# Attention and two feed-forward layers on one core: who splits w_in, and where tile 2's w_in products stand in the second step

## The chip, the core and the metric

The kernel runs on one core of one Trainium2 chip. The metric is the device time of one execution in microseconds (us), the median of several runs. In the profile PE is TensorE, DVE is VectorE, ACT is ScalarE, POOL is GpSimd and SP is SyncE, whose queue issues nearly all DMAs.

## The reference

Three layers follow each other on 1536 rows (2 batches of 768) of width 512 (8 heads of 64):

```python
# attention, per batch and head: 768 queries, the last 128 keys and 4 sink keys
scores = q @ k.T / 8
keep   = (key < 4) | ((0 <= query - key) & (query - key < 128))
x      = softmax(where(keep, scores, -1e9)) @ v          # heads side by side: [1536, 512]

# first layer, d_ff = 1024
h    = x @ w_in
solu = h * softmax(h)
ln   = (solu - mean(solu)) / sqrt(var(solu) + 1e-6) * g_ln
x    = ln @ w_out

# second layer, d_ff = 2048
y = relu(x @ w2_in) ** 2 @ w2_out
```

## The kernel before

**Numbers in two parts.** A product of two f32 matrices is made of three products of a rounded type (fp32r). Each operand is rounded ("hi"), what the rounding lost is kept as a second operand ("lo"), and PE sums hi x hi, hi x lo and lo x hi. So every matrix that PE multiplies is first rounded by one engine and split (raw minus hi) by one. For w_in these are `round_w_in(c)` and `split_w_in(c)` for its 4 chunks of 128 rows (128x1024 each, in w_raw, w_hi, w_lo); for w_out `round_w_out(first, last)` on ACT and `split_w_out(first, last)` on DVE for the 8 chunks of 128x512 (wo_hi, wo_lo), with the layernorm's gain g_col multiplied in. `WO_POOL` names the w_out chunks that POOL does all by itself (`split_w_out(i, k)`, three instructions), `WO_DVE` the others.

**Stage A** goes over 12 tiles of 128 rows (`NT`), in a software pipeline written out by hand: each engine has a function `step(t)` that lists its instructions in order, and the engines wait for each other's semaphores. In step t PE does the values of tile t+1 (`values`, `sink_values`: probabilities times v, in o_ps), the transposes of tile t's normalised hidden rows (`transpose_ln(t)`), the scores of tile t+2 (`score(t + 2, p)`, p = 0 to 3 for four pairs of heads), the w_in products of tile t+1 (`hidden(t + 1, first, last)`, 24 matmuls of 128x512 in h_ps), the w_out products of tile t (`project(t, first, last)`, 24 matmuls), and the transposes of probabilities (`transpose_p`, `transpose_sinks`) and of tile t-1's result (`transpose_x2`). Around them ACT copies and rounds from PSUM, and makes the exponentials (`softmax_exp`, `hidden_exp`); DVE masks (`merge`), takes the row maxima (`row_max`, `hidden_max`), normalises (`normalize_p`), gates and measures (`gate_and_norm`: u = h * e, bn_stats, variance), normalises the hidden rows (`normalize_hidden`) and makes the low parts (`split_xT`, `split_lnT`, `split_k`, `split_q`); POOL computes the inverse deviation (`inverse_std`), zeroes the triangular halves of the transposed probabilities (`halves`) that `values` reads, rounds the sink probabilities (`gather_sinks`) and prepares the sinks' values (`build_v_sink`, `split_v_sink`).

**The first tiles** are special, since all of w_in and w_out has to be split while they run. Tile 0's w_in products go by chunk: `hidden_0(c, False)` needs w_hi only, `hidden_0(c, True)` needs w_lo as well. `first_step()` is step 0; its w_out products are `project_0(with_low, first, last)`. Step 1 is `step(1)` with exceptions: `project_0(True, 3, C1)` for tile 0 and the scores of tile 3 stand ahead of `transpose_ln(1)`. `ln_parts(t)` says in which PSUM banks the transposes of the layernorm land: for tile 0 in w1_ps and o_ps, for all others in w1_ps and the two banks of h_ps, so that `hidden(t + 1, ...)` has to wait until these are read. `keep_warm` issues matmuls whose result is not used.

**Stage B** (from about 250 us) is the second layer in 3 blocks of 512 rows (`hidden2`, `project2`). Its weights are loaded over w_in's and w_out's raw copies: SP's queue waits for w_split, w_split_pool, wo_split and wo_split_pool ahead of the first such load (L372 to L376).

Of the kernel before, what the change touches and what calls it, by code (L numbers as in the profile page):

```python
# [27 lines left out]
NT = BATCH * TPB  # L28
# [7 lines left out]
WO_POOL = (6, 7)  # L36
# [93 lines left out]
def attention_moe_program(nc, qT, kT, v, w_in, w_out, g_ln, w2_in, w2_out, out):  # L130
# [6 lines left out]
    with ctx:  # L137
# [174 lines left out]
        def _(sp):  # L312
# [55 lines left out]
            for n in range(3, NT):  # L368
# [33 lines left out]
        def _(pool):  # L402
# [67 lines left out]

            def split_v_sink(b):

                low = slice(2 * SK, SKS)
                nc.gpsimd.tensor_copy(v_sink[0:SKS, b, :], v_sink_raw[0:SKS, b, :]).then_inc(v_sink_step, 1)
                pool.wait_ge(v_sink_step, 2 * b + 2)
# [24 lines left out]
            pool.wait_ge(w_rounded, 1)  # L500
            for half in range(2):
                cols = slice(half * BANK, (half + 1) * BANK)
                nc.gpsimd.tensor_tensor(w_lo[:, 0, cols], w_raw[:, 0, cols], w_hi[:, 0, cols].bitcast(F32), ALU.subtract
                                        ).then_inc(w_split_pool, 1)
            build_v_sink(0)
            split_v_sink(0)
# [34 lines left out]
        def _(act):  # L541
# [87 lines left out]
            def step(t, nxt=True):  # L629
# [3 lines left out]
                if t > 1:  # L633
                    copy_x2(t - 1)
                if t > 1 and t + 3 < NT:
                    round_q(t + 3)
                round_xT(n)
                if t == 1:
                    copy_x2(0)
                round_lnT(t)  # L640
                if t == 1:
                    round_q(4)
                if nxt:
# [9 lines left out]
                    bias(t + 2, 1)  # L653
                    if t + 3 < NT:
                        round_k(t + 3)
                    for h in range(HG, H):
                        softmax_exp(t + 2, h)
                    hidden_exp(n)
                    copy_pT(t + 2, 0)
                    copy_x2T(t - 1)  # L660
                    copy_pT(t + 2, 1)
                    if has_sinks(t + 2):
                        copy_sinksT(t + 2)

            def first_step():
# [4 lines left out]
                round_w_out(3, len(WO_DVE))  # L670
# [5 lines left out]
                round_lnT(0)  # L676
                bias(2, 1)
# [16 lines left out]

            bias(0, 0)
# [19 lines left out]
            copy_pT(1, 1)  # L715
            copy_sinksT(1)
# [664 lines left out]
```

## Time and profile before

| | us |
|---|---|
| runs (3) | 513.96, 513.05, 513.89 |
| median | 513.89 |
| profiled execution, time | 512.32 |
| profiled execution, span | 510.6 |
| PE busy | 493.1 (97%) |
| DVE busy | 281.1 (55%) |
| ACT busy | 212.2 (42%) |
| POOL busy | 103.6 (20%) |

The span is the time from the first to the last profiled instruction; the time of the same execution is 1.72 us longer. The profiled execution was not the median one. PE's clock has two levels, 1.2 and 2.4 GHz; "granted clock 0.50" in a stretch means that it ran at 1.2 GHz all along, 1.00 that it ran at 2.4.

### The profile page before, as it was taken

What the parts mean: (1) busy time and instruction counts of PE and PEld (TensorE: products, weight loads), DVE (VectorE), ACT (ScalarE), POOL (GpSimd) and SP (SyncE); (2) the same over time, 40 slices, a digit from 0 to 9 for tenths busy, and PEclk for the clock granted to TensorE, in tenths of its full rate; (3) what the DMA queues carried; (4) which work ended last, traced back from release to release, by engine and by line L of the source; (5) the groups of instructions that cost most, each with busy time, mean ns of one, the idle gap of its engine ahead of it and who ended that gap; (6) DMA issues with size and microseconds to landing.
All of it is one profiled execution on the core that took longest, in us unless ns stands there. A gap on an engine that the chain in (4) does not pass through costs nothing.

```text
span 510.6 us, 7209 instructions
## 1 busy us (share of the span) xinstructions
PE 493.1 (97%) x2676; PEld 400.1 (78%) x2676; DVE 281.1 (55%) x501; ACT 212.2 (42%) x556; POOL 103.6 (20%) x139
## 2 busy tenths in 40 slices
PE   7977899999999999999999999999999999999997
PEld 5656687888788888878877888888888888888885
DVE  3989688787788787674689334333222223222222
ACT  3756176565666656553354233232122122121121
POOL 4436204220021122072997000000000000000000
PEclk9999699999999999999999999999999999999999
DMA  8820312323121020006200000020000002000002
GB/s 248 279 64 21 126 43 104 114 74 122 46 61 45 22 62 1 22 1 225 105 0 1 1 0 1 0 82 0 0 0 0 0 0 83 0 1 0 1 0 83
DMA packets 12837, 26.04 MB, mean 51 GB/s; under 512 B 1608, under 2 KB 2632, under 8 KB 12296
## 3 DMA queue, kind: packets, MB, share of 16 engines
q1 hardware_dynamic: 12504, 25.39, 15.4%
q8 instruction: 18, 0.29, 0.2%
q10 hardware_dynamic: 304, 0.27, 0.2%
q14 instruction: 11, 0.09, 0.1%
HBM read 22.51 MB, written 3.15 MB: 50 GB/s over the span
## 4 chain that ended last, share of the span: by engine, by line
PE 86%; DVE 7%; ACT 3%; DMA 1%; issue 1%; POOL 1%; SPq 0%; DVEq 0%; POOLq 0%
PE score_ps L1306 25%; PE h_ps L1318 12%; PE w_ps L1165 12%; PE h_ps L1127 12%; PE wt_ps L1318 6%; PE w_ps L1318 6%; PE o_ps L1097 3%; PE score_ps L1068 2%; ACT prob L574 2%; PE wt_ps L1075 2%; PE wt_ps L1068 1%; PE h_ps L1155 1%; PE o_ps L1193 1%; DMA w2in<-w_in 1%; PE o_ps L1114 1%
## 5 line engine op out<-in xcount | busy, mean ns | idle before, releaser
L1306 PE MATMUL score_ps<-x2T_hi,w2in_hi 128*128 (+1 forms) x192 | 74.9, 390 | 0.0
L1306 PE MATMUL score_ps<-x2T_hi,w2in_lo 128*128 (+1 forms) x192 | 74.7, 389 | 0.0
L1306 PE MATMUL score_ps<-x2T_lo,w2in_hi 128*128 (+1 forms) x192 | 74.7, 389 | 0.0
L1005 DVE TENSOR_TENSOR e<-e 128x512 f32<-128x512 f32 x24 | 18.5, 771 | 81.7 <-ACT e L744 81.7
L1005 DVE TENSOR_TENSOR sq<-relu 128x512 f32<-128x512 f32 x24 | 17.5, 728 | 80.5 <-ACT relu L744 80.5
L744 ACT ACTIVATE relu<-score_ps 128x512 f32<-128x512 f32 x24 | 14.4, 598 | 92.1 <-PE score_ps L1306 92.1
L744 ACT ACTIVATE e<-score_ps 128x512 f32<-128x512 f32 x24 | 14.4, 600 | 87.4 <-PE score_ps L1306 87.3
L1306 PEld LDWEIGHTS score_ps<-x2T_lo,w2in_hi 128*128 128x128 f32 x192 | 36.1, 188 | 7.4
L1306 PEld LDWEIGHTS score_ps<-x2T_hi,w2in_hi 128*128 128x128 f32 x192 | 36.0, 188 | 7.5
L1306 PEld LDWEIGHTS score_ps<-x2T_hi,w2in_lo 128*128 128x128 f32 x192 | 36.0, 188 | 7.4
L574 ACT ACTIVATE prob<-sm,nbias 128x132 f32<-128x132 f32 (+1 forms) x96 | 37.9, 396 | 0.5
L1127 PE MATMUL h_ps<-w_hi,xT_hi 128*128 128x512 f32 x88 | 35.6, 404 | 1.8 <-DVE xT_lo L881 1.8
L1165 PE MATMUL w_ps<-wo_hi,lnT_hi 128*128 128x512 f32 x88 | 35.8, 407 | 1.2 <-DVE lnT_lo L876 1.1
L1165 PE MATMUL w_ps<-wo_lo,lnT_hi 128*128 128x512 f32 x88 | 35.3, 401 | 0.0
L1165 PE MATMUL w_ps<-wo_hi,lnT_lo 128*128 128x512 f32 x88 | 34.4, 391 | 0.0
L1127 PE MATMUL h_ps<-w_hi,xT_lo 128*128 128x512 f32 x88 | 34.4, 390 | 0.0
L1127 PE MATMUL h_ps<-w_lo,xT_hi 128*128 128x512 f32 x88 | 34.3, 390 | 0.0
L426 POOL CAST p_sink<-prob 128x64 fp32r<-128x64 f32 x10 | 3.8, 381 | 115.0 <-DVE prob L869 104.1
L536 POOL TENSOR_TENSOR w2in_lo<-w2in,w2in_hi 128x512 fp32r<-128x512 f32 x16 | 25.6, 1599 | 1.3
L593 ACT ACTIVATE e<-h_ps,nhmax 128x512 f32<-128x512 f32 x24 | 16.3, 685 | 22.6 <-DVE nhmax L821 22.6
L1127 PEld LDWEIGHTS h_ps<-w_hi,xT_hi 128*128 128x128 f32 x88 | 16.5, 188 | 6.4 <-issue 2.0
L1165 PEld LDWEIGHTS w_ps<-wo_hi,lnT_hi 128*128 128x128 f32 x88 | 16.6, 189 | 5.9 <-DVE lnT_lo L876 1.8
(178 smaller groups left out, 1143.9 us busy)
## 6 DMA issues: line engine op xcount, KB each, us to landing
w2in<-w_in SPq DMA_DIRECT2D x4, 1024.0 KB, 5.2
w2out<-w_out SPq DMA_DIRECT2D x8, 512.0 KB, 7.5
V<-v SPq DMA_DIRECT2D x12, 256.0 KB, 2.7
k_raw<-kT SPq DMA_DIRECT2D x20, 132.0 KB, 2.8
q_raw<-qT SPq DMA_DIRECT2D x20, 128.0 KB, 2.8
w2in<-w_in SPq DMA_DIRECT2D x4, 512.0 KB, 6.1
w2in<-w_out SPq DMA_DIRECT2D x2, 1024.0 KB, 10.8
out<-u SPq DMA_DIRECT2D x6, 256.0 KB, 2.0
```

Source lines behind the costliest of these rows:

```text
L536: nc.gpsimd.tensor_tensor(w2in_lo[:, :, fs], w2in[:, :, fs], w2in_hi[:, :, fs].bitcast(F32), ALU.subtract).then_inc(w2in_split, 1)
L574: nc.scalar.activation(prob[:, h, seen(n)], sm[:, h, seen(n)], ACT.Exp, bias=nbias[:, h:h + 1], scale=SCALE, accum_out=psum_row[:, h:h + 1 ...
L593: nc.scalar.activation(e[:, cols], h_ps[:, cols], ACT.Exp, bias=nhmax[:, :], scale=1.0, accum_out=hsum[:, half:half + 1]).then_inc(h_exped, 1)
L744: nc.scalar.activation(relu[f % 2], h2_ps[f % 2], ACT.Relu).then_inc(relu_ready, 1)
L1005: nc.vector.tensor_tensor(sq[f % 2], relu[f % 2], relu[f % 2], ALU.mult).then_inc(sq_ready, 1)
L1068: done = mm(bank, qs[rows], ks[rows], start=(i == 0), stop=(i == len(products) - 1))
L1075: last = nc.tensor.transpose(pT_ps[g][:, j * P:(j + 1) * P], prob[:, g * HG + j, main(n)], ident[:, :])
L1097: last = mm(o_ps[rows, cols], V[:, slot, h * D:(h + 1) * D], pT[:, g, j * P:(j + 1) * P], start=(g == 0 and part == 0 and i < 2), stop=(al ...
L1127: done = mm(h_ps[:, cols], xs[:, c, :], ws[:, c, cols], start=(c == 0 and k == 0), stop=(c == MC - 1 and k == 2))
L1165: done = mm(x2_ps[:, :], ls[:, k, :], ws[:, k, :], start=(k == 0 and i == 0), stop=(k == C1 - 1 and i == 2))
L1306: done = mm(h2_ps[f % 2], ws[:, c, fs], xs[:, c, bass.ts(blk, BLK)], start=(c == 0 and i == 0), stop=(c == MC - 1 and i == 2))
L1318: done = mm(y_ps[q], gs[f % 2][:, qs], ws[:, f, :], start=(f == 0 and i == 0), stop=(f == C2 - 1 and i == 2))
```

## The change

- `split_w_in`: POOL makes the low parts of chunks 0, 2 and 3 (before: 0), DVE that of chunk 1 (before: 1, 2, 3). `round_w_in(0)` goes from DVE to ACT. The low part of v_sink for batch 0 goes from POOL to DVE.
- `WO_POOL` is (7,), before (6, 7): chunk 6 of w_out is rounded by ACT and split by DVE.
- Tile 1's layernorm is transposed into w1_ps and o_ps as well (`EARLY = 2`), and PE's second step is written out: tile 2's w_in products stand ahead of `transpose_ln(1)`, with `project_0(True, 2, C1)` between them; 16 w_out products stand between the scores and the transposes of tile 3.
- The order of the first two steps of ACT and DVE is changed: among others, one w_out chunk instead of three is rounded ahead of `round_xT(1)`, `split_xT(1)` stands between the two `stats(0, ...)`, `normalize_p(2, 1)` ahead of `hidden_max(1, ...)`, and `split_w_out(2, 7)` ahead of `normalize_hidden(1)`. On PE `hidden_0(2, True)` and `hidden_0(3, True)` go ahead of `transpose_p(1, 0)`; 3 `keep_warm` products remain 3, in two places.

```diff
-WO_POOL = (6, 7)
+WO_POOL = (7,)
+EARLY = 2
 ln_parts(t):
-            if t == 0:
+            if t < EARLY:
                 return [(0, 4, w1_ps[:, :], 2), (4, C1, o_ps[:, :], 1)]
 SP, ahead of the first load of w2_in:
-                    sp.wait_ge(w_split, MC - 1)
-                    sp.wait_ge(w_split_pool, 2)
+                    sp.wait_ge(w_split, 1)
+                    sp.wait_ge(w_split_pool, 2 * (MC - 1))
 POOL:
-            pool.wait_ge(w_rounded, 1)
-            for half in range(2):
-                ...
+            def split_w_in(c):
+                pool.wait_ge(*((w_rounded, 2) if c == 2 else (w_rounded_act, c // 3 + 1)))
+                for half in range(2):
+                    ...
+            split_w_in(0)
             build_v_sink(0)
-            split_v_sink(0)
+            round_v_sink(0)
+            split_w_in(2)
+            split_w_in(3)
             round_q(2)
             round_k(2)
             halves(1, 0)
 ACT:
+            round_w_in(0)
             bias(0, 0)
...
+            hidden_exp(0)
             copy_sinksT(1)
-            hidden_exp(0)
             act.wait_ge(g_loaded, 16)
-            round_w_out(0, 3)
+            round_w_out(0, 1)
             first_step()
-            for t in range(1, NT - 2):
+            second_step()
+            for t in range(EARLY, NT - 2):
 ACT first_step():
-                round_w_out(3, len(WO_DVE))
+                round_w_out(1, 5)
...
                 round_lnT(0)
+                round_w_out(5, len(WO_DVE))
                 bias(2, 1)
...
-                hidden_exp(1)
                 copy_pT(2, 0)
                 copy_pT(2, 1)
+                hidden_exp(1)
                 copy_sinksT(2)
+            def second_step():                     # ACT
+                round_xT(2)
+                copy_earlier(3, 0)
+                copy_earlier(3, 1)
+                round_q(4)
+                copy_x2(0)
+                bias(3, 0)
+                softmax_exp(3, 0)
+                softmax_exp(3, 1)
+                round_lnT(1)
+                copy_earlier(3, 2)
+                copy_earlier(3, 3)
+                softmax_exp(3, 2)
+                softmax_exp(3, 3)
+                finish(1)      # bias(3,1), round_k(4), 4 exponentials, hidden_exp(2), copies: as in step()
 DVE:
-            round_w_in(0)
             merge(0, 1)
...
+            round_w_in(2)
             split_w_in(1)
-            round_w_in(2)
...
             row_max(1, 0)
+            split_v_sink(0)
             merge(1, 3)
...
             normalize_p(1, 1)
-            split_w_in(2)
-            split_w_in(3)
             hidden_max(0, 0)
...
-            gate_and_norm(0)
             first_step()
 DVE first_step():
+                gate(0, 0)
+                gate(0, 1)
+                stats(0, 0)
+                split_xT(1)
+                stats(0, 1)
+                variance(0)
                 merge(2, 0)
                 merge(2, 1)
                 normalize_hidden(0)
                 row_max(2, 0)
-                split_w_out(0, 1)
                 merge(2, 2)
                 merge(2, 3)
                 row_max(2, 1)
+                split_w_out(0, 1)
                 for part in range(2):
                     split_lnT(0, part)
-                split_w_out(1, 2)
                 normalize_p(2, 0)
                 split_q(3)
+                split_w_out(1, 2)
+                normalize_p(2, 1)
                 hidden_max(1, 0)
                 hidden_max(1, 1)
                 hidden_max_all(1)
-                normalize_p(2, 1)
-                split_w_out(2, 3)
-                gate_and_norm(1)
                 split_k(3)
+            def second_step():                     # DVE
+                gate(1, 0)
+                gate(1, 1)
+                stats(1, 0)
+                stats(1, 1)
+                variance(1)
+                split_xT(2)
+                split_w_out(2, len(WO_DVE))
+                normalize_hidden(1)
+                merge(3, 0)
+                merge(3, 1)
+                row_max(3, 0)
+                for part in range(2):
+                    split_lnT(1, part)
+                merge(3, 2)
+                merge(3, 3)
+                row_max(3, 1)
+                normalize_p(3, 0)
+                split_k(4)
+                split_q(4)
+                hidden_max(2, 0)
+                hidden_max(2, 1)
+                hidden_max_all(2)
+                normalize_p(3, 1)
+                gate_and_norm(2)
 PE:
             hidden_0(0, True)
             hidden_0(1, True)
-            transpose_p(1, 0)
-            keep_warm(3)
-            transpose_p(1, 1)
             hidden_0(2, True)
             hidden_0(3, True)
+            transpose_p(1, 0)
+            keep_warm(1)
+            transpose_p(1, 1)
+            keep_warm(2)
             first_step()                           # its last project_0(True, 0, 3) is (True, 0, 2)
+            def second_step():                     # PE
+                values(2, 0)
+                values(2, 1)
+                sink_values(2)
+                score(3, 0)
+                score(3, 1)
+                pe.wait_ge(u_ready, 3)
+                hidden(2, 0, 12)
+                pe.wait_ge(u_ready, 4)
+                hidden(2, 12, 16)
+                project_0(True, 2, C1)
+                hidden(2, 16, 24)
+                transpose_ln(1)
+                score(3, 2)
+                score(3, 3)
+                project(1, 0, 16)
+                transpose_p(3, 0)
+                transpose_x2(0)
+                transpose_p(3, 1)
+                transpose_sinks(3)
+                project(1, 16, 24)
```

## Rows read from the trace of the kernel before

**Rows 1.** The page, part 2: granted TensorE clock in tenths, 40 slices of 12.8 us

```profile
PEclk9999699999999999999999999999999999999999
```

**Rows 2.** Windows: stretch, us, busy us of each engine (instructions), PEclk, DMA

```profile
51.80:66.80 15.00, 12.76 (x81) 9.83 (x80) 9.19 (x20) 3.90 (x9) 2.58 (x4) 0.70 0.33 107
...
77.80:250.00 172.20, 170.92 (x1173) 140.35 (x1173) 129.22 (x274) 98.89 (x310) 45.61 (x70) 1.00 0.23 75
```

**Rows 3.** Windows of the same form around the low clock

```profile
26.00:28.00 2.00, 0.73 (x2) 0.30 (x2) 2.00 (x2) 0.36 (x1) 2.00 (x2) 1.00 0.00 0
50.50:54.00 3.50, 3.50 (x27) 2.76 (x27) 3.25 (x9) 1.00 (x3) 2.78 (x6) 0.51 0.02 5
57.70:64.20 6.50, 6.50 (x27) 4.62 (x28) 1.90 (x4) 1.57 (x4) 0.00 (x0) 0.50 0.55 193
```

**Rows 4.** Timeline of PE: start, us, operation, [idle before <- releaser]

```profile
12.43 0.66 PE L1075 MATMUL wt_ps<-ident,prob 128*128 128x128 f32 x4 [1.02 <-DVE prob L869]
...
22.63 1.07 PE L1144 MATMUL h_ps<-w_lo,xT_hi 128*128 128x512 f32 x4
...
26.68 0.73 PE L1144 MATMUL h_ps<-w_lo,xT_hi 128*128 128x512 f32 x2 [0.95 <-DVE w_lo L941]
28.25 0.73 PE L1144 MATMUL h_ps<-w_lo,xT_hi 128*128 128x512 f32 x2 [0.84 <-DVE w_lo L941]
...
35.08 0.47 PE L1127 MATMUL h_ps<-w_hi,xT_hi 128*128 128x512 f32 x1 [1.82 <-DVE xT_lo L881]
...
46.28 0.50 PE L1183 MATMUL w_ps<-wo_hi,lnT_hi 128*128 128x512 f32 x1 [0.25 <-POOL wo_lo L497]
...
49.87 0.66 PE L1075 MATMUL wt_ps<-ident,prob 128*128 128x128 f32 x4 [2.37 <-DVE prob L869]
...
57.48 2.98 PE L1183 MATMUL w_ps<-wo_lo,lnT_hi 128*128 128x512 f32 x5 [2.07 <-DVE wo_lo L887]
...
65.91 0.39 PE L1068 MATMUL score_ps<-KH,QH 64*128 64x260 f32 x2 [0.16 <-DVE sm L799]
...
77.81 0.66 PE L1097 MATMUL o_ps<-pT_own,V 128*64 128x128 f32 x8
```

**Rows 5.** Timeline of DVE, in the same form

```profile
7.30 0.69 DVE L946 TENSOR_SCALAR w_hi<-w2in 128x1024 fp32r<-128x1024 f32 x1 [7.30 <-DMA w2in<-w_in]
...
24.94 3.26 DVE L941 TENSOR_TENSOR w_lo<-w2in,w_hi 128x1024 fp32r<-128x1024 f32 x2
...
56.68 2.07 DVE L887 SCALAR_TENSOR_TENSOR wo_lo<-w2in,g_col,wo_hi 128x512 fp32r<-128x512 f32 x3
...
73.81 0.71 DVE L869 TENSOR_TENSOR prob<-prob,rz 128x528 f32<-128x528 f32 x1
```

**Rows 6.** Timeline of ACT, in the same form

```profile
18.18 1.06 ACT L688 ACTIVATE w_hi<-w2in 128x1024 fp32r<-128x1024 f32 x1
...
31.79 1.94 ACT L626 ACTIVATE wo_hi<-w2in,g_col 128x512 fp32r<-128x512 f32 x3
33.63 0.58 ACT L609 ACTIVATE xT_hi<-o_ps 128x512 fp32r<-128x512 f32 x1
```

**Rows 7.** Timeline of POOL, in the same form

```profile
8.14 2.54 POOL L503 TENSOR_TENSOR w_lo<-w2in,w_hi 128x512 fp32r<-128x512 f32 x2 [4.20 <-DVE w_hi L946]
14.25 1.94 POOL L468 TENSOR_TENSOR v_sink_raw<-v_sink_raw,own_head 96x512 f32<-96x512 f32 x1 [3.56 <-DMA v_sink_raw<-v]
...
24.91 0.65 POOL L436 TENSOR_SCALAR_AFFINE_SELECT pT_own<-pT_earlier 128x512 f32<-128x512 f32 x1 [1.97 <-ACT pT_earlier L579]
...
27.07 1.22 POOL L426 CAST p_sink<-prob 128x64 fp32r<-128x64 f32 x1
...
93.16 0.24 POOL L426 CAST p_sink<-prob 128x64 fp32r<-128x64 f32 x1 [10.96 <-issue]
```

**Rows 8.** The chain that ended last, pieces: start, us, what

```profile
66.88 5.69 PE h_ps L1127 x24
...
74.61 0.44 PE wt_ps L1075 x4
```

More of the change, by code:

```diff
@@ L652, in step, with finish @@
                     softmax_exp(t + 2, 3)
[L653 to L663, printed above, removed]
+                    finish(t)
+            def finish(t):
+                bias(t + 2, 1)
+                if t + 3 < NT:
+                    round_k(t + 3)
+                for h in range(HG, H):
+                    softmax_exp(t + 2, h)
+                hidden_exp(t + 1)
+                copy_pT(t + 2, 0)
+                copy_x2T(t - 1)
+                copy_pT(t + 2, 1)
+                if has_sinks(t + 2):
+                    copy_sinksT(t + 2)
             def first_step():
@@ L821, in hidden_max_all, with gate, stats, variance @@
                 nc.vector.tensor_reduce(nhmax[:, :], hmax[:, :], AX_X, ALU.max, negate=True).then_inc(hmax_ready, 1)
[L823 to L834 removed]
+            def gate(t, half):
+                cols = slice(half * BANK, (half + 1) * BANK)
+                dve.wait_ge(h_exped, 2 * t + half + 1)
+                nc.vector.tensor_tensor(u[:, cols], h_ps[:, cols], e[:, cols], ALU.mult).then_inc(u_ready, 1)
+                if half == 1:
+                    nc.vector.scalar_tensor_tensor(hz[:, :], hsum[:, 0:1], SM_EPS, hsum[:, 1:2], ALU.add,
+                                                   ALU.add).then_inc(hz_ready, 1)
+            def stats(t, half):
+                dve.wait_ge(u_ready, 2 * t + half + 1)
+                nc.vector.bn_stats(bstat[:, half, :], u[:, half * BANK:(half + 1) * BANK]).then_inc(bstat_ready, 1)
+            def variance(t):
                 dve.wait_ge(hz_ready, t + 1)
@@ L842, in gate_and_norm @@
                 nc.vector.tensor_tensor(var[:, :], moments[:, 1:2], hz_eps[:, :], ALU.add).then_inc(var_ready, 1)
+            def gate_and_norm(t):
+                for half in range(2):
+                    gate(t, half)
+                    stats(t, half)
+                variance(t)
             def normalize_hidden(t):
@@ L882, in split_xT, with split_v_sink @@
                                         xT_hi[:, :, :].bitcast(F32), ALU.subtract).then_inc(xT_split, 1)
+            def split_v_sink(b):
+                low = slice(2 * SK, SKS)
+                dve.wait_ge(v_sink_step, 2 * b + 2)
+                nc.vector.tensor_tensor(v_sink[low, b, :], v_sink_raw[low, b, :], v_sink[low, b, :].bitcast(F32),
+                                        ALU.subtract).then_inc(v_sink_ready, 1)
             def split_w_out(first, last):
@@ L974, in _ @@
             split_q(2)
-            gate_and_norm(0)
             first_step()
-            for t in range(1, NT - 2):
+            second_step()
+            for t in range(EARLY, NT - 2):
                 step(t)
@@ L1207, in step @@
                     sink_values(n)
-                if t == 1:
-                    project_0(True, 3, C1)
-                    score(3, 0)
-                    score(3, 1)
-                elif nxt and alone(n):
+                if nxt and alone(n):
                     score(t + 2, 0)
@@ L1215, in step @@
                 transpose_ln(t)
-                if nxt and not alone(n) and t > 1:
+                if nxt and not alone(n):
                     score(t + 2, 0)
@@ L1282, in _ @@
             hidden_0(1, True)
-            transpose_p(1, 0)
-            keep_warm(3)
-            transpose_p(1, 1)
             hidden_0(2, True)
             hidden_0(3, True)
+            transpose_p(1, 0)
+            keep_warm(1)
+            transpose_p(1, 1)
+            keep_warm(2)
             first_step()
-            for t in range(1, NT - 2):
+            second_step()
+            for t in range(EARLY, NT - 2):
                 step(t)
```

43 lines of the change are left out of this document (13 added, 30 removed).

## Prediction

> **What bounds the kernel now.** I read TensorE's (PE's) granted clock in the page's 40 slices first: it is full but for the fifth slice, 51 to 64 us, with 6 tenths [rows 1]. The windows then separate two regimes: from 77.8 to 250 us PE is busy 170.92 of 172.20 us, so there everything else is hidden; from 51.8 to 66.8 it is busy only 12.76 of 15.00 us and at a mean clock of 0.70 [rows 2]. An edit that touches tiles 0 to 2 is therefore worth what it takes out ahead of 77.81 us, where PE begins the values of tile 3 [rows 4]; behind that point the same instructions follow and the saving should be carried to the end unchanged.
>
> Ahead of it PE's own timeline gives the waits: 0.95 and 0.84 us for DVE's low parts of w_in, 1.82 for xT_lo of tile 1, 0.25 for POOL's low part of w_out, 2.37 for DVE's normalised probabilities, 2.07 for DVE's low parts of w_out and 0.16 for a merge [rows 4]. Two stretches ran at the lower level, 1.2 of 2.4 GHz: 50.5 to 54.0 (clock 0.51) and 57.7 to 64.2 (clock 0.50) [rows 3]. Each follows a wait, the one of 2.37 and the one of 2.07 us. The waits of 0.95, 0.84 and 1.82 us were followed by no fall; 26 to 28 us shows 0.73 us of work in 2.00 at a clock of 1.00 [rows 3].
>
> **The front: up to the first w_in product of tile 1.** Before it starts at 35.08 [rows 4]. Four edits meet here.
>
> First, ACT instead of DVE rounds chunk 0 of w_in. DVE began with that rounding, 0.69 us from 7.30 [rows 5], and its first merge stood behind it, although PE's scores were there by then. DVE gains up to 0.7 us; ACT has nothing to do until the first row maxima, and its own rounding of such a chunk took 1.06 [rows 6], so it is done at about 8.4, ahead of the maxima at 8.6. PE had waited 1.02 us before the transposes at 12.43 [rows 4], so up to 0.76 can come through. After that ACT, PE and DVE hand over to each other with little slack; I take 0.6, bounds 0 and 0.76.
>
> Second, DVE loses the two low parts of w_in (3.26 us at 24.94 [rows 5]) and POOL gets them: four halves of 128x512 at 1.27 us each by the pair at 8.14 [rows 7]. POOL's queue there is: multiply of v_sink at 14.25 after its load lands (1.94), its rounding (0.95), and then the halves, from about 17.2. Uncontended they end at 22.3. Behind them in POOL's queue stand the rounding of q and k of tile 2 (0.6 each) and the triangular halves of tile 1, which PE's values wait for. DVE meanwhile runs about three passes of 0.7 us over two SBUF tensors; if POOL loses that time, the end is 24.4. I take 23.5. PE asks for the last low part at 22.63 (where its low products began [rows 4]) less 0.6, plus six products of 0.24, or 23.4. So the waits of 0.95 and 0.84 go, and PE has all of h of tile 0 at about 23.9, not at 28.9.
>
> What is late next is POOL: rounding q and k until about 24.7, then the halves of tile 1. Before, that group held a p_sink cast of 1.22 us at 27.07 where the same cast took 0.24 at 93.16 [rows 7]; DVE was just then in its w_lo passes. Those are gone, so from 25.0, when ACT has copied the first transposes, I take four selects of 0.65 (the one at 24.91 [rows 7]) and two short steps, 3.3 us, plus 0.3 for the DVE passes that come nearer: done at 28.6. Bounds 27.9 and 30. PE then has half of the values and the sinks left, 1.1 us, to 29.75; scores of tile 2 run to 30.7.
>
> Here the Trainium skill, GPSIMD Engine Reference, section 1 (Specifications), speaks against the change: GpSimd shares its SBUF interfaces with VectorE and contends with VectorE instructions that read two SBUF inputs or run in a 2-port mode. By that rule the low parts would stretch over DVE's passes and end at 24.4 instead of 22.3; the sum with either would differ by about 1 us. By that rule, the trace agrees: 1.22 against 0.24 us for one cast [rows 7].
>
> Third, ACT rounds one chunk of w_out there, not three. Three took 1.94 us from 31.79 and held xT_hi of tile 1 until 33.63 [rows 6]; now it follows the sinks at once. xT_hi 29.85 to 30.4 (0.58 [rows 6]), xT_lo to 31.1 (0.7, as DVE's pass of about this size at 73.81 [rows 5]), first w_in product at 31.3. The six other chunks go later on ACT, in the place where it used to wait; each costs 0.65 by the three in 1.94. Fourth, DVE gets the v_sink low part, 0.7 us, in a place where it waited for ACT; POOL loses a whole chunk of w_out later. Landmark one: **35.08 - 31.3 = 3.8 us gained**, bounds 0.6 (POOL slow, below) and 4.6.
>
> **The middle: up to the values of tile 3.** From 35.08 to 77.81 before is 42.73 us. Idle in it: 0.25 + 2.37 + 2.07 + 0.16 = 4.85 [rows 4]. The lower clock: half of 3.5 and of 6.5 us, 5.0 [rows 3]. PE's work at full clock is thus 42.7 - 4.85 - 5.0 = 32.9 us, and the change neither adds nor removes any there. What waits will it have?
>
> (a) The 2.37 us wait: tile 2's second normalisation now stands ahead of the row maxima of h and behind one w_out pass. The exponentials end near 41.4, the probabilities at 42.75; PE arrives at 43.3. Gone. POOL's selects for the values of tile 2, four of 0.65 us [rows 7], are next and leave PE about 0.9 us in pieces. Bounds 0 and 2.6.
>
> (b) The 2.07 us wait: DVE still has five low parts of w_out (0.7 each by the three from 56.68 [rows 5]) when tile 2's values end, but PE now runs sixteen w_in products first, 16 x 0.237 = 3.8 us by the 24 in 5.69 [rows 8], which covers them. That is possible because the layernorm's transposes now go to the two banks that h does not use. The w_in products in turn wait for xT_hi and xT_lo of tile 2: 0.58 + 0.7 plus signals is 1.5 us, of which the first scores of tile 3 cover 0.97 (from 65.91 [rows 4] to 66.88 [rows 8]); DVE comes to it behind the gate and moments of tile 1. I take 0.9, bounds 0.5 and the old 1.82.
>
> (c) A new wait. In the old second step 24 w_in products stood between the last scores of tile 3 and the transposes of its probabilities. Now only sixteen w_out products (3.8) and two groups of transposes (0.44 each [rows 8]) do, so PE is through 0.97 + 3.8 + 0.88 = 5.6 us after starting those scores. From those scores to the normalised probabilities took 65.91 to 74.52 before, 8.6 us [rows 4, 5]. Some of ACT's exponentials are now done ahead of them, some layernorm roundings stand in front; bounds 7.0 and 8.6, I take 7.8. **PE waits 2.2 us**, bounds 1.4 and 3.0. Queued behind the waiting transpose are the sink transpose, the last eight w_out products and the values of tile 3.
>
> So the middle takes 32.9 + 0.9 + 0.9 + 2.2 = 36.9 us, **5.8 us gained**, and both together 9.6 us, if the clock stays up. The wait (c) is as long as the two that were followed by a fall. One such stretch costs 1.7 (3.5 us at half) to 3.25 us (6.5 at half); I take 2.4. In the case without a fall PE comes to the transposes of tile 2's layernorm early and waits there some 0.5 us for POOL's root and DVE.
>
> **Hidden edits.** DVE's total falls (3.26 + 0.69 off, 0.7 + 0.7 on); ACT's added w_in and w_out chunks lie under PE's w_in products of tile 1; if the cover is gone the w_out chunks cost 0.65 each. The loads hang on the splits of q and k and on the values, which all move forward, and no DMA is added. SP's wait ahead of the first big w2_in load names other semaphores, but the last to come is still DVE's w_out, some 6 us earlier; q and k of tile 5 queue behind it and are not needed for 15 us.
>
> **The sum.** The profiled execution has a span of 510.6 and a time of 512.32; the median of the three runs is 513.89, 1.57 above it. I subtract from the median: 9.6 - 2.4 = 7.2, so 506.7.
>
> **Rivals.**
> 1. No fall at (c), or one that other waits swallow: 9.6 - 0.5 = 9.1, so 504.8. For it: 1.82 us was followed by none, and PE is dense before the wait. Against it: both waits above 2 us were.
> 2. GpSimd becomes the bound in front. If its four halves are slowed as the v_sink multiply seems to be (1.94 us for 96 rows, longer than a 128-row half), by about 1.6, the last ends near 26 and the triangular halves near 31.6: 3 us late, 4.2 gained, 509.7 (507.5 without a fall). Against it: DVE reads PSUM in half of its passes there.
> 3. Handovers are each late, with a second fall after (a) and (b), as in the old order: 9.6 - 2.4 - 3, so 509.3.
> 4. Nothing: POOL's work replaces DVE's one for one and the new wait the old ones; 513.9. The profile speaks against it, since at least the 1.94 us of w_out roundings leave the chain.
> 5. Slower: after wait (c) the clock does not come back. Each us at half costs 0.5, so 9.6 us are eaten only by 19 us at the lower level; a whole step more (18.5 + 6.5 us) would give 12.5 - 9.6 = 2.9 more, 516.8. The longest stretch seen was 6.5 us and the steps from 77.8 on have no wait to start one.
>
> **Numbers.** Forecast 44% (its own range 505.5 to 508.2), rival 1 24%, rival 2 15%, rival 3 10%, rival 4 3%, rival 5 4%. The range 503.8 to 510.3 leaves out rivals 4 and 5 and some of the tails. Runs of this kernel tell 0.2%, about 1.0 us, from no change: faster 0.93, same 0.03, slower 0.04.
>
> **What would show it.** Right: no wait of PE on w_lo; its first w_in product of tile 1 near 31.3; h of tile 2 begun before the layernorm's transposes; a single wait over 2 us, on DVE's probabilities in the second step, with a clock near 0.5 behind it; the values of tile 3 near 70. Wrong: POOL's low parts past 24.4 with PE waiting on them, waits on POOL's selects over 1.5 us, or a changed length of the part from there to the end.

## The result and the profile after

The changed kernel takes 506.27 us (median of 4 runs, 504.81 to 507.02) against 513.47 (4 runs, 512.58 to 513.96): ratio 0.9858, 95% interval 0.9829 to 0.9888. That is 7.2 us less, as forecast to the tenth (506.7 from 513.89). The sum agrees, its terms do not: the front gave half of its 3.8 us or less, and the low clock stretch, for which 2.4 us had been taken off, cost about 0.3. The two profiled executions are only 5.3 us apart (512.32 and 507.02): that of the kernel before lies 1.57 below the median that the prediction started from, that of the changed kernel 0.75 above its own.

The profiled execution took 507.02 with a span of 505.3. These are PE's waits in it (start, us, operation, idle before and what ended it), the same places as [rows 4] and the new ones:

```profile
12.92 0.66 PE L1143 MATMUL wt_ps<-ident,prob 128*128 128x128 f32 x4 [2.14 <-DVE prob L904]
...
23.62 2.04 PE L1212 MATMUL h_ps<-w_lo,xT_hi 128*128 128x512 f32 x8
27.10 0.66 PE L1143 MATMUL wt_ps<-ident,prob 128*128 128x128 f32 x4 [1.44 <-DVE prob L904]
...
31.17 0.31 PE L1173 MATMUL score_ps<-ident,p_sink 128*96 128x128 f32 x1 [0.65 <-POOL p_sink L430]
...
35.21 0.47 PE L1195 MATMUL h_ps<-w_hi,xT_hi 128*128 128x512 f32 x1 [0.58 <-DVE xT_lo L916]
...
48.53 0.66 PE L1165 MATMUL o_ps<-pT_own,V 128*64 128x128 f32 x8 [0.48 <-POOL pT_own L437]
...
53.19 0.47 PE L1195 MATMUL h_ps<-w_hi,xT_hi 128*128 128x512 f32 x1 [0.58 <-DVE xT_lo L916]
...
62.24 0.50 PE L1233 MATMUL w_ps<-wo_hi,lnT_hi 128*128 128x512 f32 x1 [0.18 <-DVE lnT_lo L911]
...
68.93 0.66 PE L1143 MATMUL wt_ps<-ident,prob 128*128 128x128 f32 x4 [1.88 <-DVE prob L904]
...
72.98 0.86 PE L1165 MATMUL o_ps<-pT_own,V 128*64 128x128 f32 x8
...
75.59 0.40 PE L1223 MATMUL w_ps<-ident,u 128*128 128x128 f32 x2
```

The first w_in product of tile 1 starts at 35.21; it was 35.08 [rows 4] and the forecast said 31.3. From there to the values of tile 3 it is 37.77 us (72.98 - 35.21), where 42.73 had been. The sign "the values of tile 3 near 70" is missed. Up to 35.21 the waits for w_in's low parts (0.95 and 0.84) are gone: the eight products at 23.62 follow each other. But then PE waits 1.44 us for the probabilities of tile 1 and 0.65 for POOL's. Behind 35.21 the waits are 0.48 on POOL (forecast 0.9 in pieces), 0.58 on xT_lo (0.9), 0.18, and the new one of 1.88 (2.2), in the place that step (c) named.

What held the probabilities back stands in DVE's timeline of the changed kernel:

```profile
15.91 0.69 DVE L1016 TENSOR_SCALAR w_hi<-w2in 128x1024 fp32r<-128x1024 f32 x1 [1.43 <-DMA w2in<-w_in]
...
19.66 1.06 DVE L833 COPY_PREDICATED sm<-sink_is_key,never 128x16 f32<-128x16 uint32 x1
...
22.86 0.81 DVE L833 COPY_PREDICATED sm<-sink_is_key,never 128x16 f32<-128x16 uint32 x1
...
25.37 0.57 DVE L899 TENSOR_SCALAR z_eps<-psum_row 128x4 f32<-128x4 f32 x1
```

The same short steps in DVE's timeline of the kernel before:

```profile
18.66 0.61 DVE L805 COPY_PREDICATED sm<-sink_is_key,never 128x16 f32<-128x16 uint32 x1
...
20.64 0.17 DVE L805 COPY_PREDICATED sm<-sink_is_key,never 128x16 f32<-128x16 uint32 x1
...
22.11 0.17 DVE L864 TENSOR_SCALAR z_eps<-psum_row 128x4 f32<-128x4 f32 x1
```

POOL's timeline of the changed kernel at that time:

```profile
17.16 1.48 POOL L469 TENSOR_TENSOR v_sink_raw<-v_sink_raw,own_head 96x512 f32<-96x512 f32 x1 [5.26 <-DMA v_sink_raw<-v]
...
19.39 5.50 POOL L508 TENSOR_TENSOR w_lo<-w2in,w_hi 128x512 fp32r<-128x512 f32 x4
```

And ACT's, where the load of chunk 0 is first used:

```profile
8.18 1.06 ACT L714 ACTIVATE w_hi<-w2in 128x1024 fp32r<-128x1024 f32 x1 [4.20 <-DMA w2in<-w_in]
```

The load of chunk 0 was there at 8.18 (7.30 before [rows 5]), DVE waited 1.43 us for chunk 2 although the low part of chunk 1 behind it in its order was ready to be made, and v_sink's load came at 17.16 (14.25 before [rows 7]). POOL's four halves run from 19.39 to 24.89, past the prediction's mark of 24.4, but PE did not wait for them. In that time a DVE copy of 16 columns takes 1.06 us and its twin 0.81 (0.61 and 0.17 before), and z_eps, four numbers per row, takes 0.57 beside POOL's next cast, which starts at 24.83 (0.17 before).

The windows around the new wait, and of the rest of stage A (us, busy us of PE, PEld, DVE, ACT and POOL, granted clock, DMA share, GB/s):

```profile
66.90:69.00 2.10, 0.22 (x3) 0.07 (x2) 2.00 (x7) 1.13 (x3) 0.06 (x1) 1.00 0.37 119
70.00:71.00 1.00, 1.00 (x4) 0.81 (x3) 1.00 (x3) 0.93 (x3) 0.93 (x2) 0.52 0.22 76
71.00:72.00 1.00, 1.00 (x4) 0.72 (x3) 0.89 (x3) 0.00 (x0) 0.93 (x3) 0.50 0.00 0
72.00:73.00 1.00, 1.00 (x5) 0.35 (x3) 0.79 (x3) 0.00 (x0) 0.52 (x2) 0.50 0.00 0
73.00:245.00 172.00, 170.83 (x1173) 140.59 (x1173) 128.65 (x273) 98.67 (x311) 45.16 (x69) 1.00 0.23 75
```

The granted clock falls from 1.00 to half speed (the 1.2 GHz level of the two) after the wait, as forecast, and is back at 2.4 GHz at about 73.4, after some 3.4 us. From 73 us on PE is busy 170.83 of 172.00 us, as [rows 2] had it: the gain of stage A's start is carried to the end.

### The profile page after: what moved, and what is told of

It reads as the page before. It is cut to its first block, busy times and chain, and to the rows that moved or that the text cites. A ratio compares the mean times of both kernels' runs of the same rounds, so it can differ in the third digit from the quotient of the medians.

```text
span 505.3 us, 7210 instructions
## 1 busy us (share of the span) xinstructions
PE 489.4 (97%) x2676; PEld 398.1 (79%) x2676; DVE 277.7 (55%) x499; ACT 213.6 (42%) x557; POOL 101.6 (20%) x139
## 4 chain that ended last, share of the span: by engine, by line
PE 88%; DVE 6%; DMA 2%; SPq 1%; ACT 1%; issue 1%; POOL 1%; DVEq 0%; ACTq 0%
PE score_ps L1395 25%; PE h_ps L1407 12%; PE h_ps L1195 12%; PE w_ps L1233 12%; PE wt_ps L1407 6%; PE w_ps L1407 6%; PE o_ps L1165 4%; PE score_ps L1136 2%; PE wt_ps L1143 2%; DMA w2in<-w_in 2%; PE wt_ps L1136 1%; PE o_ps L1182 1%; PE h_ps L1223 1%; PE o_ps L1261 1%; PE w_ps L1251 1%
## 5 line engine op out<-in xcount | busy, mean ns | idle before, releaser
L1195 PE MATMUL h_ps<-w_hi,xT_lo 128*128 128x512 f32 x88 | 34.3, 390 | 0.0
L1195 PE MATMUL h_ps<-w_lo,xT_hi 128*128 128x512 f32 x88 | 34.3, 390 | 0.0
## 6 DMA issues: line engine op xcount, KB each, us to landing
w2out<-w_out SPq DMA_DIRECT2D x8, 512.0 KB, 7.2
w2in<-w_in SPq DMA_DIRECT2D x4, 512.0 KB, 7.8
```

What stands on the lines that cost most here:

```text
L1195: done = mm(h_ps[:, cols], xs[:, c, :], ws[:, c, cols], start=(c == 0 and k == 0), stop=(c == MC - 1 and k == 2))
```

## The experiments

All are built from the changed kernel unless it is said otherwise. The kernel before had a median of 513.59 in the first two groups (11 and 15 runs) and 513.93 in the last (11 runs). The mean clock of a run, given below for some, is the granted clock over the whole execution: one stretch of 3.4 us at half speed makes it 0.997, none 1.00.

**The changed kernel again.** No edit.

> The changed kernel once more, for a second profile. In its first profile w_in's chunk 0 reached ACT at 8.18 us (7.30 reached DVE before), chunk 2 kept DVE waiting 1.43 us and v_sink's load kept POOL until 17.16 (14.25 before). If the front's missing gain (first w_in product of tile 1 at 35.21, forecast 31.3) is an accident of that execution's loads, this profile has the loads at about 7.3 and 14.3 and that product at 31 to 33. If it is built into the new order, the product is again near 35. Time 506.3 either way.

506.41 us (6 runs, 505.75 to 506.70), and again a first product near 35:

```profile
34.92 0.47 PE L1195 MATMUL h_ps<-w_hi,xT_hi 128*128 128x512 f32 x1 [0.59 <-DVE xT_lo L916]
...
68.66 0.66 PE L1143 MATMUL wt_ps<-ident,prob 128*128 128x128 f32 x4 [1.85 <-DVE prob L904]
...
71.40 0.66 PE L1165 MATMUL o_ps<-pT_own,V 128*64 128x128 f32 x8
...
74.71 0.41 PE L1223 MATMUL w_ps<-ident,u 128*128 128x128 f32 x2 [0.75 <-DVE u L883]
```

The loads were late once more (chunk 0 at 7.94, 1.34 us of waiting for chunk 2), so the front's missing gain is no accident of one execution. And this execution had no low clock: the values of tile 3 start 36.48 us after the first product instead of 37.77, 1.3 earlier. But 0.75 of that is spent waiting for DVE's u at the layernorm's transposes, which start 39.79 us after the first product here and 40.38 in the profile above. So what the low stretch cost this pair is 0.6 us at the transposes and only 0.3 one step later: the scores behind them start 41.04 us after the first product here (75.96) and 41.37 in the profile above (76.58). The times of the runs give little more: of the six those with a mean clock of 1.00 took 506.40, 505.75 and 506.61, those with 0.997 took 506.43, 506.22 and 506.70. (Of the result's own four runs the one at 1.00 took 504.81 and the three at 0.997 took 505.71, 506.84 and 507.02; that hints at more, but it rests on one run, and the six here do not repeat it.)

Six profiles of this study have the same second step and a wait of 1.85 to 1.90 us at this place. From the transposes behind the wait to the end of the span, the four in which the clock fell afterwards took 436.2 to 436.5 us, the two in which it did not 436.0 and 436.1. The stretch costs the end about 0.3 us.

**Only the front undone.**

```diff
-            round_w_in(0)          # ACT; DVE has it again
 POOL:
-            round_v_sink(0); split_w_in(2); split_w_in(3)
+            split_v_sink(0)
 DVE:
+            split_w_in(2); split_w_in(3)      # behind normalize_p(1, 1)
...
 PE:
-            hidden_0(2, True); hidden_0(3, True); transpose_p(1, 0); keep_warm(1); transpose_p(1, 1); keep_warm(2)
+            transpose_p(1, 0); keep_warm(3); transpose_p(1, 1); hidden_0(2, True); hidden_0(3, True)
 ACT:
-            round_w_out(0, 1)
+            round_w_out(0, 3)
...
```

Not shown: DVE's old order of w_in's low part 1 and the rounding of chunk 2, of v_sink and of tile 0's moments, and ACT's of hidden_exp(0), are restored too.

> The changed kernel with only its front put back to the old order: DVE rounds chunk 0 and makes w_in's low parts 1, 2 and 3, POOL makes v_sink's low part, PE transposes tile 1's probabilities before the last two low products, ACT rounds three w_out chunks ahead of xT_hi. The second step stays new. The prediction's theory (front worth 3.8 us): 3.8 slower than the changed kernel, about 510. Rival, from the profile after (front worth nothing, all of the gain in the second step): the same as the changed kernel, 506.3 within 0.7.

507.90 us (507.08 to 508.15). The front is worth 1.5 us here, between the two theories, and nearer to the rival. The old waits are back in PE's timeline:

```profile
26.71 0.73 PE L1211 MATMUL h_ps<-w_lo,xT_hi 128*128 128x512 f32 x2 [0.95 <-DVE w_lo L1008]
28.29 1.05 PE L1211 MATMUL h_ps<-w_lo,xT_hi 128*128 128x512 f32 x2 [0.84 <-DVE w_lo L1008]
...
36.45 0.47 PE L1194 MATMUL h_ps<-w_hi,xT_hi 128*128 128x512 f32 x1 [1.63 <-DVE xT_lo L913]
```

With them the granted clock is below full in the third slice of the page, 25.3 to 38.0 us, and the window shows where:

```profile
PEclk9989999999999999999999999999999999999999
...
28.50:32.00 3.50, 3.50 (x21) 2.26 (x20) 2.66 (x5) 0.35 (x2) 1.40 (x3) 0.51 0.00 0
```

This pair of profiles tells something that the profile of the kernel before hid. That one has the same waits of 0.95 and 0.84 us at the same times within 0.04, with the first load as early (7.30 and 7.33 us), but no fall behind them, and its first product starts at 35.08 instead of 36.45. So a low stretch here costs 1.3 us at that product, not 0.3. Against 36.45 the changed kernel's 35.21 is 1.2 us earlier; against 35.08 it is no gain at all. How often the kernel before falls there can only be guessed from its runs. Its profiled execution has a mean clock of 0.990, from the two stretches of [rows 3]; of its 37 runs here 19 have 0.983 to 0.987, so at least one stretch more, with a median of 514.72, and the other 18 have 513.07. No profile of one of the 19 is kept, so that the further stretch lies in the front is not shown. Nor do the six runs above settle it: the two with the fullest clock took 507.76 (1.00) and 507.08 (0.999), the others 507.82 to 508.15.

The second step alone is worth 513.59 - 507.90 = 5.7 us.

**Products that keep PE busy in the new wait.**

```diff
                 transpose_x2(0)
+                warm_tr(7)       # 7 products of 128x512 into the bank of the next transposes
                 transpose_p(3, 1)
```

> The changed kernel with 7 more products whose result is not used, 128x512, in the wait of 1.88 us ahead of the second transposes of tile 3's probabilities. Theory that the wait lets the clock fall (3.1 us at 0.5 in the profile after) and that this costs the end: no low stretch, values of tile 3 about 1.5 earlier, time 1.2 to 1.7 below the changed kernel, about 504.8. Rival, the waits behind it (POOL's selects, the layernorm) swallow the low stretch: the same, 506.3. Third case, the products themselves delay PE by up to 0.5.

506.54 us (505.89 to 508.33): the rival, no gain. The seven products do their work: the wait is down to 0.26, and the granted clock is 1.00 over the eight w_out products behind it, from 71.24 on:

```profile
68.43 1.84 PE L1270 MATMUL wt_ps<-lnT_lo 128*128 128x512 f32 x7
70.53 0.66 PE L1143 MATMUL wt_ps<-ident,prob 128*128 128x128 f32 x4 [0.26 <-DVE prob L904]
```

That fits the 0.3 us of the six profiles above, which is less than these times can tell. (The profiled execution was the slowest of the six: it waited 1.65 us for a merge at 19.70 and had a low stretch there, from about 19.8 to 23.2.)

**Row maxima of h earlier.**

```diff
                 row_max(3, 0)
+                hidden_max(2, 0)
+                hidden_max(2, 1)
+                hidden_max_all(2)
                 for part in range(2):
                     split_lnT(1, part)
...
                 split_q(4)
-                hidden_max(2, 0)
-                hidden_max(2, 1)
-                hidden_max_all(2)
                 normalize_p(3, 1)
```

> The changed kernel with DVE's three row maxima of tile 2's h moved to the 2.80 us in which DVE waits for ACT's layernorm rounding, so that they no longer stand ahead of the normalisation of tile 3's second half. Theory that this chain sets PE's wait: 1.88 falls to 0.6 or less, no low clock stretch, 1.3 + 1.5 gained, about 503.5. Rival: PE gains the wait but loses it again at the values of tile 3 (POOL) or at the layernorm's transposes, 505.5 to 506.3.

504.63 us (503.49 to 505.38), 1.8 below the changed kernel and between the two expectations. The wait of 1.88 is 0.67 here, and 0.49 remains at the layernorm's transposes:

```profile
67.76 0.66 PE L1143 MATMUL wt_ps<-ident,prob 128*128 128x128 f32 x4 [0.67 <-DVE prob L904]
...
73.53 0.41 PE L1223 MATMUL w_ps<-ident,u 128*128 128x128 f32 x2 [0.49 <-DVE u L883]
```

So it was DVE's order that made wait (c) so long. Shortening it brought 1.2 us there; the values of tile 3 start 35.2 us after the first product (70.48 - 35.26), and the clock does not fall.

**Two orders of DVE in the front.**

```diff
-            round_w_in(2)
             split_w_in(1)
+            round_w_in(2)
...
             row_max(1, 0)
-            split_v_sink(0)
             merge(1, 3)
...
             hidden_max_all(0)
+            split_v_sink(0)
```

> The changed kernel with two orders of DVE in the front altered: w_in's low part 1 ahead of the rounding of chunk 2 (DVE waited 1.43 and 1.34 us there for the load with that low part ready to be made), and v_sink's low part behind the row maxima of tile 0's h instead of ahead of tile 1's last merge (where the second row maxima came 1.0 us after ACT was free for them). Theory that these two waits are what ate the front's forecast gain: the first w_in product of tile 1 goes from 35 to about 33.5, time 1.0 to 1.8 lower, about 504.8. Rival, the front is held by POOL's queue (low parts until 24.6, selects of tile 1): within 0.4 of the changed kernel, 506.4.

505.78 us (505.17 to 505.98), 0.6 lower, less than the theory's 1.0 to 1.8 and hardly more than the rival's 0.4. In the profile the wait for the probabilities shrinks from 1.44 to 0.28 and the first product starts at 33.98:

```profile
26.49 0.66 PE L1143 MATMUL wt_ps<-ident,prob 128*128 128x128 f32 x4 [0.28 <-DVE prob L904]
...
33.98 0.47 PE L1195 MATMUL h_ps<-w_hi,xT_hi 128*128 128x512 f32 x1 [0.59 <-DVE xT_lo L916]
```

Part of that is luck: chunk 0 was there at 7.43 in this execution, by ACT's timeline:

```profile
7.43 1.06 ACT L714 ACTIVATE w_hi<-w2in 128x1024 fp32r<-128x1024 f32 x1 [3.46 <-DMA w2in<-w_in]
```

Its runs with clock 0.997 (505.98, 505.17) lie on both sides of those with 1.00 (505.29 to 505.83).

**The rounding of chunk 0 back on DVE.**

```diff
 ACT:
-            round_w_in(0)
             bias(0, 0)
 DVE:
+            round_w_in(0)
             merge(0, 1)
```

> The changed kernel with only the rounding of w_in's chunk 0 back on DVE. In four profiles with it on ACT the chunk reached the engine at 7.9 to 8.7 us, in the two profiles with it on DVE at 7.30 and 7.33. Theory that ACT's taking it is the cause of the late loads: the chunk is there at 7.3 again, DVE does not wait for chunk 2, time 0.5 to 1.0 lower. Rival, the loads vary by themselves or with something else in the front: late in this one too, and the time the same or up to 0.7 higher (DVE's first merge stands behind the rounding again).

507.04 us (506.58 to 507.70), 0.6 slower. In time that edit is worth what the prediction gave it, but the profile does not show the gain where it was forecast. With the same load time as in the repeated profile the first product starts earlier here, at 34.43 instead of 34.92, and PE then waits 0.90 us instead of 0.48 for POOL:

```profile
34.43 0.47 PE L1195 MATMUL h_ps<-w_hi,xT_hi 128*128 128x512 f32 x1 [0.59 <-DVE xT_lo L915]
...
48.17 0.66 PE L1165 MATMUL o_ps<-pT_own,V 128*64 128x128 f32 x8 [0.90 <-POOL pT_own L437]
```

Where the 0.6 us are lost stays open. The theory that ACT's taking it is what delays the loads finds no support: the chunk came late with DVE too, at 7.96.

```profile
7.96 0.69 DVE L1015 TENSOR_SCALAR w_hi<-w2in 128x1024 fp32r<-128x1024 f32 x1 [7.96 <-DMA w2in<-w_in]
```

Over all twelve profiles of this study the engine that rounds chunk 0 starts at 7.30, 7.33, 7.43, 7.84, 7.94, 7.96, 8.18, 8.40, 8.46, 8.66, 8.84 and 9.28 us, with the same loads in the same order. The kernel before, with 7.30, was at the early end. The three with DVE are 7.30, 7.33 and 7.96, all in the earlier half, so twelve profiles do not rule that theory out either.

**The front alone, on the kernel before.** The front's edits on the kernel before; the order of tile 0's moments, the row work of tile 2, the second step and POOL's two w_out chunks are the old ones.

```diff
 POOL:
-            split_v_sink(0)
+            round_v_sink(0); split_w_in(2); split_w_in(3)
 ACT:
+            round_w_in(0)
             bias(0, 0)
...
-            round_w_out(0, 3)
+            round_w_out(0, 1)
 DVE:
-            round_w_in(0)
...
+            split_v_sink(0)           # behind row_max(1, 0)
...
-            split_w_in(2); split_w_in(3)
 PE:
+            hidden_0(2, True); hidden_0(3, True)
             transpose_p(1, 0); keep_warm(1); transpose_p(1, 1); keep_warm(2)
```

> The kernel before with the new front only (w_in's low parts, the rounding of chunk 0, v_sink's low part, the order of PE's low products, one w_out chunk ahead of xT_hi; the gate's order is the old one), the old second step and two w_out chunks on POOL. Theory that the two halves of the change add up: as much below the kernel before as undoing the front cost, 1.5, so 512.1, and the second step is worth 5.6. Rival 1 (the prediction's terms): 3.8 below, 509.8. Rival 2: the front's gain is only there with the new second step, 513.6.

511.67 us (10 runs, 510.54 to 513.27), 1.9 below the kernel before. With 5.7 for the second step this makes 7.6, where both together gave 7.2: they add up. None of the ten runs has a mean clock below 0.989, where 19 of the 37 of the kernel before have: by its runs, the new front takes away a low stretch that the old kernel often had, and part of the 1.9 us goes with it. Its six runs at 0.990 have a median of 512.0, the fourteen of the kernel before at 0.990 512.8; at equal clock 0.8 us is left. The old waits of 2.37 and 2.07 us are still there, as 1.80 and 2.07:

```profile
36.06 0.47 PE L1141 MATMUL h_ps<-w_hi,xT_hi 128*128 128x512 f32 x1 [0.59 <-DVE xT_lo L891]
...
50.65 1.11 PE L1089 MATMUL wt_ps<-ident,prob 128*128 128x128 f32 x4 [1.80 <-DVE prob L879]
...
59.52 0.49 PE L1197 MATMUL w_ps<-wo_lo,lnT_hi 128*128 128x512 f32 x1 [2.07 <-DVE wo_lo L903]
```

**Both improvements together.** The diffs of the early row maxima and of the two orders of DVE, both applied.

> The early row maxima of tile 2's h (504.63 alone) and the two altered orders of DVE together. If what they shorten lies in series: 504.6 less 1.0 to 1.8, about 503.2. If POOL holds the front: 504.6.

504.00 us (503.42 to 505.76), between the two expectations, ratio to the kernel before 0.9806, interval 0.9777 to 0.9836. The best of the study, 2.4 us below the changed kernel, although its profiled execution had the latest load of all:

```profile
9.28 1.06 ACT L714 ACTIVATE w_hi<-w2in 128x1024 fp32r<-128x1024 f32 x1 [5.30 <-DMA w2in<-w_in]
```

**Without GpSimd's two low parts.** Zeros are put there at the start, while POOL is idle; the low part of half of w_in is left out.

```diff
+            for c in (2, 3):                   # at about 2.7 to 5 us
+                for half in range(2):
+                    nc.gpsimd.tensor_copy(w_lo[:, c, cols], zeros ...).then_inc(w_split_pool, 1)
...
             round_v_sink(0)
-            split_w_in(2)
-            split_w_in(3)
```

> The changed kernel without the four GpSimd subtractions that make w_in's low parts 2 and 3: in their place GpSimd copies zeros there at the start, from about 3 to 6 us, where it is idle, and PE's products with them are kept. So part of the computation (the low part of half of w_in) is left out. Theory that these subtractions cost the front twice, by POOL's lateness and by slowing DVE's short steps meanwhile (two copies of 16 columns took 1.06 and 0.81 us against 0.61 and 0.17 before, z_eps 0.57 against 0.17): the two copies are back near 0.2 to 0.6, the probabilities of tile 1 two us earlier, the first w_in product of tile 1 near 33, time 1.5 to 2 below the changed kernel, 504.5 to 505. Rival, only the order of DVE and ACT holds the front: within 0.4 of 506.4.

505.27 us (504.40 to 506.77), 1.1 lower, less than the 1.5 to 2 expected. The two short copies are down to 0.17 us each, PE does not wait for tile 1's probabilities at all, and the first product starts 2.3 us earlier than in the repeated profile (34.92 - 32.62). Not all of that is the subtractions': the first of the two copies starts 0.8 us earlier already (18.56, there 19.37), in an execution in which chunk 2 kept DVE waiting for 0.51 us and not 1.34. The 1.5 us that are left agree better with the times. DVE's timeline:

```profile
18.56 0.17 DVE L836 COPY_PREDICATED sm<-sink_is_key,never 128x16 f32<-128x16 uint32 x1
...
20.68 0.17 DVE L836 COPY_PREDICATED sm<-sink_is_key,never 128x16 f32<-128x16 uint32 x1
```

PE's:

```profile
32.62 0.47 PE L1198 MATMUL h_ps<-w_hi,xT_hi 128*128 128x512 f32 x1 [0.59 <-DVE xT_lo L919]
```

32.62 is what the front gave in one execution with none of POOL's four subtractions, still 1.3 us short of the forecast's 31.3.

**Chunk 3's low part on DVE**, on top of the best kernel.

```diff
 POOL:
             split_w_in(2)
-            split_w_in(3)
 DVE:
             normalize_p(1, 1)
+            split_w_in(3)
 PE:
             hidden_0(2, True)
-            hidden_0(3, True)
             transpose_p(1, 0)
             keep_warm(1)
             transpose_p(1, 1)
+            hidden_0(3, True)
```

> The best kernel so far (early row maxima and the two altered orders, 504.0) with the low part of chunk 3 back on DVE, behind tile 1's normalisations, and PE's products with it behind the transposes of tile 1's probabilities. If POOL's second pair of halves disturbs DVE by about 1 us: DVE pays 1.2 to 1.6 us for that low part itself, at a place where PE waits for POOL's selects; between 0.5 faster and 0.5 slower, 503.5 to 504.5. Rival, tile 0's row maxima of h move back by the whole low part and the gate, xT_lo and the first w_in product with them: 1.2 slower, 505.2.

504.90 us (503.65 to 507.35), 0.9 above the best kernel, between the two expectations, with ranges that overlap. PE now waits for that low part and, three times as long, for xT_lo (0.58 in the best kernel's profile):

```profile
26.89 0.73 PE L1212 MATMUL h_ps<-w_lo,xT_hi 128*128 128x512 f32 x2 [0.48 <-DVE w_lo L1010]
...
33.95 0.47 PE L1195 MATMUL h_ps<-w_hi,xT_hi 128*128 128x512 f32 x1 [1.55 <-DVE xT_lo L915]
```

POOL's second pair of halves disturbs DVE, but by these medians not more than the pass would cost DVE itself. The runs differ with the clock: the three at 1.00 took 503.65, 504.30 and 504.33, as fast as the best kernel, the two at 0.997 505.47 and 505.97 and the one at 0.993 507.35. In the profile, one of those at 0.997, the low stretch stands behind the wait of 1.55, from about 34.3 to 37.7 us. Whether the stretch costs the time or longer waits cost both is not separated by this.

## Why the prediction was right, and where it was not

**The place of the gain: right.** Between the two profiles 4.8 of the 5.3 us lie ahead of tile 3's values (77.81 and 72.98), and the rest of stage A is as dense as it was: 170.83 of 172.00 us busy. Steps (a) and (b) hold: the waits of 2.37 and 2.07 us are gone, with 0.48 on POOL's selects (0.9 forecast) and 0.58 on xT_lo (0.9 forecast) in their place. Undoing the front leaves 5.7 us of gain; the forecast's middle was 5.8 before the clock.

**Step (c), the new wait: right** in place, releaser and size (1.88 and 1.85 against 2.2). Moving DVE's row maxima out of its chain took 1.2 us off it, which shows that its place in the chain sets most of the wait; the other 0.67 us stay.

**"One such stretch costs 1.7 to 3.25 us; I take 2.4": wrong.** The clock did fall in the profile, for 3 us. But rival 1's second half was the true account: what PE loses there it would have waited for anyway. Without the fall it waits 0.75 us for DVE and POOL at the layernorm's transposes. Measured cost: 0.3 us by the six profiles with the same wait, nothing that the runs by clock or the seven filling products can show. The price was read from the time that products take at half rate, and the wait of 0.5 us, which the prediction itself named for the case without a fall, was not taken off the case with one. The same error has another side. The prediction put no low stretch in the front, since in its one profile none followed the waits of 0.95 and 0.84 us; in the profile of the front undone one does, and there nothing behind it takes it up: 1.3 us.

**The front, "35.08 - 31.3 = 3.8 us gained": wrong in size.** It is worth 1.5 us by undoing it and 1.9 by itself, and part of that may be the low stretch just named, which the forecast's 3.8 did not count. The parts that fell short:
- The rounding on ACT did not: 0.6 forecast, 0.6 measured, though the profile does not show it ahead of the first product.
- The contention with GpSimd was charged to POOL only. POOL's four halves took 5.50 us instead of 5.08 and PE did not wait for them. DVE paid: the two copies of 16 columns 1.06 and 0.81 us against 0.61 and 0.17, tile 1's z_eps 0.57 against 0.17, in the chain that leads to tile 1's probabilities. The low parts of v_sink and k in the same chain took 1.00 and 1.12 us, against 0.68 and 0.70 without the subtractions. By leaving the subtractions out, about 1.5 us of the start of the first product came back in the profile and 1.1 us of the time. The rule that the prediction took from the Trainium skill (GPSIMD Engine Reference, section 1, Specifications) names the contention and gives it no size; the copy of 16 columns, whose mask and source both lie in SBUF, is an instruction that it names, and 0.17 against 1.06 us agrees with it. The traces show the size: the copy ends within 0.04 us of the end of a GpSimd subtraction that was running, at 22.59 and 22.56 us with the two orders altered, and at 23.79 and 23.75 us in the best kernel:

```profile
21.56 1.03 DVE L833 COPY_PREDICATED sm<-sink_is_key,never 128x16 f32<-128x16 uint32 x1
...
20.02 2.54 POOL L508 TENSOR_TENSOR w_lo<-w2in,w_hi 128x512 fp32r<-128x512 f32 x2 [0.30 <-ACT w_hi L714]
...
22.49 1.30 DVE L833 COPY_PREDICATED sm<-sink_is_key,never 128x16 f32<-128x16 uint32 x1
...
18.72 5.03 POOL L508 TENSOR_TENSOR w_lo<-w2in,w_hi 128x512 fp32r<-128x512 f32 x4 [0.69 <-DVE w_hi L1016]
```

- The order: v_sink's low part ahead of a merge was costed at nothing, because DVE waited there before, and the rounding of chunk 2 was placed ahead of a low part that was ready. Both altered, 0.6 us came back. DVE's waits there before, 0.29 and 0.40 us, were shorter than the step, forecast at 0.7 and measured at 1.00.

A further part was the base: the only profile of before had its first load at 7.30 us, the earliest of twelve, and no low stretch in the front. The 1.57 us between its time and the median, which the prediction noted and left unexplained, is about what separates the runs of the kernel before by clock (513.07 and 514.72). The forecast took its terms from a fast execution and subtracted them from a slower median.

So two errors, about 2 us too much for the front and about 2 us too much off for the clock, cancelled; that the sum came out to the tenth is luck. The range held because it allowed for both. Two of the rivals' sums do not follow from their terms: rival 2 without a fall gives 9.6 - 0.5 - 3 = 6.1 and 507.8, not 507.5, and rival 3 gives 4.2 and 509.7, not 509.3; neither decided anything.

## What to carry to other kernels

Work moved to GpSimd can be paid for by VectorE's short instructions that run beside it. Look at what stands in VectorE's chain at that time, and cost for each up to the length of the GpSimd instruction beside it (1.27 us here), not POOL's queue alone. A stretch of half clock on TensorE costs only what is not waited for afterwards: 3.4 us of it cost 0.3 us in one place of this kernel and 1.3 in another. Before charging it, find the next wait behind it. One profile gives one draw: of a load's arrival, and of whether the clock falls. Where its time lies 1.6 us below the median, ask first what the other runs have that it has not. Put the instruction that does not need the load first.

## What the runs showed of the hardware

- A VectorE copy of 128x16 takes 0.17 us alone and up to 1.30 beside GpSimd subtractions of 128x512 (1.27 each); it ends within 0.04 us of the end of one.
- The first 512 KB load of w_in, issued at the same time in the same order, was ready between 7.30 and 9.28 us in twelve executions of nearly the same program start.
- The same kernel with the same wait (1.88 and 1.85 us) had its granted clock fall to 0.5 after it in one execution and stay at 1.00 in another.
- Two executions with the same waits of 0.95 and 0.84 us ahead of the same products: the clock fell to 0.5 for 3.4 us in one and the next landmark came 1.3 us later than in the other, where it stayed at 1.00.
